# Expert products in units of 256 slots, with operands split into two fp32r parts and the second weight split during the first product

## What is computed

```python
# x: 3072 tokens of 384; w1: [8, 384, 1024]; w2: [8, 1024, 384]
do_compute = x @ w_skip > 0
xc = x[do_compute]
logits = xc @ w_gate
e_idx = np.argmax(logits, axis=1)
...
for e in range(E):
    mask = e_idx == e
    h = np.maximum(xc[mask] @ w1[e], 0.0)
    y[mask] = gate_w[mask, None] * (h @ w2[e])
out[do_compute] = xc + y
```

## Time and profile before

| | us |
|---|---|
| median of 3 runs (lowest, highest) | 1186.78 (1181.9, 1187.18) |
| profiled execution | 1180.28 |
| its span | 1178.5 |
| attention, to the first instruction of routing | about 441 |
| routing | 441 to 471 |
| experts, to the first load of `gated` | 471 to 696.6 |
| gated | 696.6 to 1178.5 |

### The profile page before, as it was taken

One profiled execution on the slowest core, in us unless ns is written; L12 is line 12 of the kernel. 1 busy time (PEld: TensorE's weight loads), 2 busy tenths in 40 slices (PEclk: granted clock), 3 DMA queues, 4 the chain that ended last, 5 costly groups with the idle time before them and its releaser, 6 DMA issues. The chain is left out here.

```text
span 1178.5 us, 23738 instructions
## 1 busy us (share of the span) xinstructions
PE 943.0 (80%) x10039; PEld 785.7 (67%) x10040; DVE 442.5 (38%) x808; ACT 282.0 (24%) x527; POOL 85.9 (7%) x113
## 2 busy tenths in 40 slices
PE   0239508885699983599999929999999999999997
PEld 0139407885688882255555518888888888888886
DVE  4762593359457117112121115542232232322322
ACT  2113202332133330011111124532323223223221
POOL 1301100102000000121112200000000000000000
PEclk9998656777589785799999968999999999999999
DMA  9203200331123115633454120001020010100101
GB/s 245 53 1 83 81 0 16 83 93 46 42 70 93 44 47 214 261 140 140 155 196 164 40 67 28 1 16 39 1 54 1 1 54 0 27 0 0 28 1 27
DMA packets 26164, 78.06 MB, mean 66 GB/s; under 512 B 4224, under 2 KB 16640, under 8 KB 23648
## 3 DMA queue, kind: packets, MB, share of 16 engines
q1 hardware_dynamic: 23904, 70.12, 18.6%
q0 software_dynamic: 2176, 6.69, 1.8%
HBM read 59.49 MB, written 17.30 MB: 65 GB/s over the span
## 5 line engine op out<-in xcount | busy, mean ns | idle before, releaser
L1212 PE MATMUL pg<-xT,wg 128*128 128x512 f32 x648 | 164.8, 398 | 1.8 <-DVE xT L1144 1.8
L1196 PE MATMUL po<-wo,hh 128*128 128x384 f32 x864 | 163.7, 337 | 0.1
L1212 PE MATMUL pv<-xT,wv 128*128 128x512 f32 x648 | 158.7, 389 | 0.0
L1196 PEld LDWEIGHTS po<-wo,hh 128*128 128x128 f32 x864 | 153.2, 188 | 5.6 <-DVE hh L1156 0.4
L1212 PEld LDWEIGHTS pv<-xT,wv 128*128 128x128 f32 x648 | 121.7, 188 | 26.2
L1212 PEld LDWEIGHTS pg<-xT,wg 128*128 128x128 f32 x648 | 121.1, 190 | 26.5 <-DVE xT L1144 3.0
L1154 DVE TENSOR_TENSOR hf<-pv,sil 128x512 f32<-128x512 f32 x72 | 49.8, 692 | 226.7 <-PE pv L1212 200.7
L940 PE MATMUL ph<-w1s,xgT 128*128 x192 | 87.8, 608 | 3.2 <-issue 3.2
L445 PE MATMUL pzx<-T,Q 32*32 32x32 f32 x768 | 16.5, 203 | 86.1 <-DVE T L363 52.9
L958 PE MATMUL py<-w2s,hT 128*128 x256 | 85.2, 486 | 0.0
L1103 ACT CAST hh<-hf 128x512 fp32r<-128x512 f32 x72 | 44.8, 622 | 151.4 <-DVE hf L1154 151.4
(11 more groups left out here) (183 smaller groups left out, 1049.2 us busy)
## 6 DMA issues: line engine op xcount, KB each, us to landing
w1s<-in_w SPq DMA_DIRECT2D x8, 1536.0 KB, 6.7
w2s<-in_w SPq DMA_DIRECT2D x8, 1536.0 KB, 10.5
kT<-in_kT SPq DMA_DIRECT2D x24, 192.0 KB, 6.2
ktok<-in_ktok SPq DMA_DIRECT2D x12, 384.0 KB, 7.4
qT<-in_qT SPq DMA_DIRECT2D x24, 192.0 KB, 3.7
vt<-in_vtok SPq DMA_DIRECT2D x12, 384.0 KB, 5.8
x_gather<-xs SPq DMA_DIRECT2D x24, 192.0 KB, 1.9
x_next<-xs SPq DMA_DIRECT2D x24, 192.0 KB, 2.0
```

The lines of the kernel that those rows point to most:

```text
L1196: ins = nc.tensor.matmul(po[j][:, 0:DM], a[:, j * 128:(j + 1) * 128], w[:, f, :], start=(f == 0 and n == 0), stop=(f == K2 - 1 and n == 2))
L1212: ins = nc.tensor.matmul(ps[:], a[:, k, c], x[:, k, :], start=(k == 0 and n == 0), stop=(k == KD - 1 and n == 2))
```

## The change

The padding is now to 256 slots, so `routing` makes units of 256 (2 tiles of gather and scatter indices each), RT is 40, and the table holds only the expert of each unit and the number of pairs of units. `experts` loops over pairs of units (10 passes at most). For each unit, whether its expert is new or not, both weights are loaded into a single buffer each and split on the chip: ACT writes `w1h[0]`, `w2h[0]` (hi), DVE writes `w1h[1]`, `w2h[1]` (lo), in halves of 1536 columns. The tokens are split into `xh`, the hidden values into `hh`. The first product has w1 as the stationary operand, so the hidden values come out with the hidden dimension on the partitions and the 8 transposes, `phT` and `hT` go. It is 72 fp32r matmuls of 256 columns; the second is 48 of 384 columns. The halves of the w2 split stand in ACT's and DVE's programs among the four groups of the first product, the split of the next unit's w1 behind the last group. `xr` goes; `yo` reads `xg`, so a gather into `xg` waits for the `yo` of the unit before the last.

```diff
--- before.py
+++ after.py
...
+UNIT = 256
+MAXU = 20
+RT = 2 * MAXU
...
-            remainder(pad[:, 1], pad[:, 0], 128)
...
+            remainder(pad[:, 1], pad[:, 0], UNIT)
...
-            for e in range(2, E):
-
-                sp.wait_ge(s_w[e % 2], 16 * NWL * (e // 2))
-                sp.wait_ge(s_y, reg(sp, TAB_ENDS + e - 2, 1, RT + 1))
...
+
+            def body(t, b, i):
+                e = reg(sp, TAB_EXPERT + t + 1, 0, E - 1)
+                sp.wait_ge(s_c1l, t + 1)
+                sp.wait_ge(s_c1h, t + 1)
+                sp.dma_start(w1s[:], w1_d[bass.ds(e, 1)].rearrange("o p n -> p (o n)")).then_inc(s_w1, 16)
+                sp.wait_ge(s_c2l, t + 1)
+                sp.wait_ge(s_c2h, t * 2 + 2)
+                sp.dma_start(w2s[:], w2_d[bass.ds(e, 1)].rearrange("o p n -> p (o n)")).then_inc(s_w2, 16)
...
             def gather(t, b):
...
+                for j in range(2):
+                    nc.gpsimd.tensor_copy(gi[b][j][:], gidx[:, bass.ds(t * 2 + j, 1)]).then_inc(s_gi, 1)
+                pool.wait_ge(s_gi, t * 2 + 2)
                 pool.sem_inc(s_step, 1)
-                nc.gpsimd.indirect_dma_start(out=xg[b][:], out_offset=None, in_=x_gather_d,
-                                             in_offset=bass.IndirectOffsetOnAxis(ap=gi[b][:, 0:1], axis=0)
-                                             ).then_inc(s_g[b], 16)
+                for j in range(2):
+                    nc.gpsimd.indirect_dma_start(out=xg[b][:, j], out_offset=None, in_=x_gather_d,
+                                                 in_offset=bass.IndirectOffsetOnAxis(ap=gi[b][j][:, 0:1], axis=0)
+                                                 ).then_inc(s_g[b], 16)
...
             def scatter(t, b, i):
...
+                for j in range(2):
+                    pool.wait_ge(s_yo, t * 2 + j + 3)
+                    pool.sem_inc(s_step, 1)
+                    nc.gpsimd.indirect_dma_start(out=x_next_d,
+                                                 out_offset=bass.IndirectOffsetOnAxis(ap=si[b][j][:, 0:1], axis=0),
+                                                 in_=yo[b][:, j], in_offset=None).then_inc(s_st[b], 16)
+
+            gather(0, 0)
+            gather(1, 1)
+
+            def body(t, b, i):
+                scatter(t, b, i)
+                gather(t + 2, b)
+                pool.wait_ge(s_st[b], i * 32 + 32)
...
-            def body(t, b, i):
-                gather(t + 2, b)
-                scatter(t, b, i)
-            pairs = tiles(pool, body)
...
+            def w1_hi(t, half):
+                c = slice(half * W1 // 2, (half + 1) * W1 // 2)
+                ins = nc.scalar.copy(w1h[0][:, c], w1s[:, c])
+                if half:
+                    ins.then_inc(s_c1h, 1)
+
+            def w2_hi(t, half):
+                c = slice(half * W2 // 2, (half + 1) * W2 // 2)
+                ins = nc.scalar.copy(w2h[0][:, c], w2s[:, c])
+                ins.then_inc(s_c2h, 1)
+
+            def x_hi(t, b):
                 act.wait_ge(s_xT, t + 1)
-                nc.scalar.copy(xgT[b][:].rearrange("p k n -> p (k n)"), pxT[:, 0:DM]).then_inc(s_xTe, 1)
+                nc.scalar.copy(xh[b][0][:, 0:2].rearrange("p k n -> p (k n)"), px[0][:])
+                nc.scalar.copy(xh[b][0][:, 2], px[1][:, 0:UNIT]).then_inc(s_xhi, 1)
 
             def body(t, b, i):
-                for f in range(2):
-                    act.wait_ge(s_h, t * 2 + f + 1)
-                    nc.scalar.activation(h[b][:, f * 512:(f + 1) * 512], ph[f][:], ACT.Relu).then_inc(s_he, 1)
+                act.wait_ge(s_w2, t * 16 + 16)
+                act.wait_ge(s_py, t * 2 + 2)
+                w2_hi(t, 0)
+                for f in range(4):
+                    act.wait_ge(s_ph, t * 4 + f + 1)
+                    nc.scalar.activation(hh[0][:, 2 * f:2 * f + 2].rearrange("p k n -> p (k n)"), ph[f][:],
+                                         ACT.Relu).then_inc(s_hhi, 1)
                     if f == 0:
-                        transposed(t + 1, 1 - b)
-            transposed(0, 0)
-            tiles(act, body)
+                        w2_hi(t, 1)
+                x_hi(t + 1, 1 - b)
+                act.wait_ge(s_w1, t * 16 + 32)
+                for half in range(2):
+                    w1_hi(t + 1, half)
+            act.sem_inc(s_py, 2)
+            act.wait_ge(s_w1, 16)
+            for half in range(2):
+                w1_hi(0, half)
+            x_hi(0, 0)
...
-            def keep(t, b, i):
-                dve.wait_ge(s_g[b], i * 16 + 16)
-
-                dve.wait_ge(s_yo, t + 1)
-                nc.vector.tensor_copy(xr[b][:], xg[b][:]).then_inc(s_xr, 1)
...
+            def w1_lo(t, half):
+                c = slice(half * W1 // 2, (half + 1) * W1 // 2)
+                ins = v.tensor_tensor(w1h[1][:, c], w1s[:, c], w1h[0][:, c].bitcast(F32), ALU.subtract)
+                if half:
+                    ins.then_inc(s_c1l, 1)
+
+            def w2_lo(t, half):
+                c = slice(half * W2 // 2, (half + 1) * W2 // 2)
+                ins = v.tensor_tensor(w2h[1][:, c], w2s[:, c], w2h[0][:, c].bitcast(F32), ALU.subtract)
+                if half:
+                    ins.then_inc(s_c2l, 1)
+
+            def x_lo(t, b):
+                dve.wait_ge(s_xhi, t + 1)
+                v.tensor_tensor(xh[b][1][:, 0:2].rearrange("p k n -> p (k n)"), px[0][:],
+                                xh[b][0][:, 0:2].rearrange("p k n -> p (k n)").bitcast(F32), ALU.subtract)
+                v.tensor_tensor(xh[b][1][:, 2], px[1][:, 0:UNIT], xh[b][0][:, 2].bitcast(F32),
+                                ALU.subtract).then_inc(s_xlo, 1)
 
             def body(t, b, i):
-                keep(t + 1, 1 - b, i + b)
-                for f in range(2):
-                    dve.wait_ge(s_hT, t * 2 + f + 1)
-                    nc.vector.tensor_copy(hT[b][:, f * 4:f * 4 + 4, :].rearrange("p k n -> p (k n)"),
-                                          phT[f][:]).then_inc(s_hTe, 1)
-
-
-                dve.wait_ge(s_y, t + 2)
-                dve.wait_ge(s_xr, t + 2)
-                nc.vector.scalar_tensor_tensor(out=yo[b][:], in0=py[b][:, 0:DM], scalar=gate[:, bass.ds(t, 1)],
-                                               in1=xr[b][:], op0=ALU.mult, op1=ALU.add).then_inc(s_yo, 1)
-            keep(0, 0, 0)
-            tiles(dve, body)
+                for f in range(4):
+                    dve.wait_ge(s_hhi, t * 4 + f + 1)
+                    k = slice(2 * f, 2 * f + 2)
+                    v.scalar_tensor_tensor(out=hh[1][:, k].rearrange("p k n -> p (k n)"), in0=ph[f][:], scalar=0.0,
+                                           in1=hh[0][:, k].rearrange("p k n -> p (k n)").bitcast(F32),
+                                           op0=ALU.max, op1=ALU.subtract).then_inc(s_hlo, 1)
+                    if f < 2:
+                        dve.wait_ge(s_c2h, t * 2 + f + 1)
+                        w2_lo(t, f)
+                x_lo(t + 1, 1 - b)
+                dve.wait_ge(s_c1h, t + 2)
+                for half in range(2):
+                    w1_lo(t + 1, half)
+                for j in range(2):
+                    dve.wait_ge(s_py, t * 2 + j + 3)
+                    dve.wait_ge(s_free, t + 1)
+                    v.scalar_tensor_tensor(out=yo[b][:, j], in0=py[j][:, 0:DM], scalar=gate[:, bass.ds(t * 2 + j, 1)],
+                                           in1=xg[b][:, j], op0=ALU.mult, op1=ALU.add).then_inc(s_yo, 1)
+            dve.wait_ge(s_c1h, 1)
+            for half in range(2):
+                w1_lo(0, half)
+            x_lo(0, 0)
+            units(dve, body)
...
             def body(t, b, i):
...
-                pe.wait_ge(s_xTe, t + 2)
-                for f in range(2):
-                    pe.wait_ge(s_he, t * 2 + f + 1)
-                    for k in range(KD):
-                        ins = nc.tensor.matmul(ph[f][:], xgT[b][:, k, :],
-                                               w1s[:, bass.ds(slot, 1), k * F1 + f * 512:k * F1 + (f + 1) * 512
...
+                pe.wait_ge(s_c1l, t + 1)
+                pe.wait_ge(s_xlo, t + 1)
+                for f in range(4):
+                    for j in range(2):
+                        m = slice((2 * f + j) * 128, (2 * f + j + 1) * 128)
+                        for k in range(KD):
+                            w = slice(k * F1 + m.start, k * F1 + m.stop)
+                            for n, (a, x) in enumerate(((0, 0), (0, 1), (1, 0))):
+                                ins = nc.tensor.matmul(ph[f][:, j * UNIT:(j + 1) * UNIT], w1h[a][:, w],
+                                                       xh[b][x][:, k], start=(k == 0 and n == 0),
+                                                       stop=(k == KD - 1 and n == 2))
+                    ins.then_inc(s_ph, 1)
                 transpose_x(t + 1, 1 - b, i + b)
-                for f in range(2):
-                    pe.wait_ge(s_he, t * 2 + f + 3)
-                    pe.wait_ge(s_hTe, t * 2 + f + 1)
```

(45 more changed lines are left out.)

164 lines of the change are left out of this document (62 added, 102 removed).

## The result

The changed kernel is **not faster but 0.9% slower**: 1193.45 us in the median (1190.92 to 1198.83, 8 runs) against 1186.58 (1178.4 to 1187.53, 8 runs), a ratio of 1.0088, 95% interval 1.006 to 1.0116. The interval excludes no change, but the difference is small, under 2%. The forecast was 1137, with a range from 1125 to 1168.

A forecast was written before the change was run, and what follows sets the result against it. PE was taken to bound the experts: first product at 490.3, 2.8 us cold and 8 units of 18.1 us brought gated 46 us earlier, giving 1134 or 1141, taken as 1137 us; range 1125 to 1168.

The forecast's parts named there:

- How many units: Experts stage: 8 units of 256 slots, one per expert, in 4 pairs, for 16 tiles before.
- PE's work in a unit: PE in the experts: a unit takes 18.1 us against 24.7 for two tiles, 53 us less for 8 units.
- rival (c): PE's 256-column matmuls: weight loads not hidden, 0.217 us per matmul, +53 us, so 1190; chance 0.05.
- The split of w1: ACT and DVE under the second product: 8.6 us plus 0.1 against 9.1 of cover, hidden by 0.4 us.
- rival (b): Split of w1: chain longer than its 0.4 us slack; 2 us more per unit is +16, 1153; chance 0.12.
- The split of w2: ACT and DVE under the first product: done at 8.2 us, PE wants it at 9.7; cost nothing.
- Ends of the stage: Experts' start and end: routing +2.5 us, first product 6.0 us later at 490.3, +1 us behind the last yo.
- the sum: Whole experts stage: the terms added up to gated at 650.5 for 696.6, 46 us less; 1137 taken.
- POOL: Gather queue: second gather issued at 4.9, landing at 8.2 us, 0.8 us before PE needs it; cost nothing.
- (a): Gathers late because DVE's w2 splits hold POOL: 1 to 2.5 us per unit, +8 to +20, up to +47; chance 0.20.

The follow-up runs named there:

- e1: Changed kernel with the xr copy back, so the gathers for unit t+2 stand ahead of the scatters of unit t; 1131.52 us.
- e10: Changed kernel with each half of DVE's w2 split as four instructions of 384 columns, same work in the same place; 1135.86 us.
- e3: Changed kernel with DVE's two halves of the w2 split behind the third and fourth hidden group instead of the first and second; 1155.21 us.
- e2: Changed kernel with SP waiting for the next unit's gathers to land before it loads the next w2; 1151.95 us.
- e7: e3 plus a spare 1.5 MB load that nobody reads, at the time of the changed kernel's w2 load; 1156.99 us.
- e4: Changed kernel with 24 filler matmuls of the identity on PE between the first product and the transposes; 1183.24 us.
- e11: Changed kernel with each half of DVE's w2 split as twelve instructions of 128 columns, same work in the same place; 1140.32 us.
- e8: e1 with gated's three 2.3 MB weight loads issued behind the w1 loads of the first two units; 1130.19 us.

## Why the prediction was wrong

**What held.** *How many units*: 8. *PE's work in a unit*: 17.6 us in e1 for 18.1; a matmul of 256 columns is 0.120 us (0.125 forecast), and rival (c), the weight loads in series at 0.217, is out. *The split of w1*: slack of 1.1 us for 0.4 (the two DVE halves took 3.4 us for 3.5, ACT's 2.9 for 3.1), so rival (b) is out. *The split of w2*: done 7.6 us into the unit for 8.2. *Ends of the stage*: from routing's start to the first product 47.4 us for 48.9 (of it routing 0.5 us more than before, forecast 2.5), from the last `yo` to `gated` 12.1 for 12.3; the cold first unit of 19.8 us is 2.2 over e1's others, for 2.8. e10, which keeps every order of the change, measures 1135.9 where the sum gave 1137; that it is so near is in part luck, since its unit of 18.1 us is 17.6 of work and 0.5 of waiting for the gathers.

**The step that failed** is *POOL*: "the second is issued at 4.9. A gather lands 3.3 us after issue in the median". The issue does start there where nothing holds it (5.2 in e3), but with DVE's splits it starts at 6.5 and ends at 8.4, and the gather is there only near 15: 8.6 us from its issue's start, for 3.3. The trace of before showed gathers only beside short DVE work; the row that spoke of long work was the earlier trace rows, and it was given to the rival.

**The rival was right in kind and mis-sized** in (a). It let POOL wait for one split; both issues are held, by 1.4 and 0.95 us. It let the second gather land at 10 to 11.5 "into the w2 load, 1 to 2.5 us late", as if landing beside the load cost little; e2 and e7 show that 2.2 us come from the hold, and 4.2 more from being issued behind the load. Its far end, "+47" from the 10.0 us landing of the earlier trace rows, came near the 6.5 us per unit, by other terms: 4.9 + 10.0 us there, 6.5 + 8.6 measured. The range left it out as the unlikely end. That row was a gather issued at 473.85, 2 us behind the last of `gated`'s three loads, and what the change made is a gather behind a large load: it was the nearest row, and the median was not.

**The term that was missing** is PE's clock. The sum priced each us of waiting as one us. The waits of 6.5 us put 1.6 us on the second product and 0.6 on the transposes: a unit is 8.7 us longer than in e1 (26.35 for 17.62), 6.5 of it waiting and 2.2 the clock; e4 gave back 2.3. Together 8.7 x 7 = 61 us, where the medians of e1 and the changed kernel lie 61.9 apart.

The Trainium skill (SBUF — State Buffer, "Who interferes with whom") has the lock for a whole instruction that the prediction set beside rival (a); the trace agrees for the gathers (1.75 us splits, 2.37 and 1.92 us issues; 1.16 with 0.5 us ones), and e11's second issue goes beyond it. The same section infers that a `tensor_tensor` leaves the generation of descriptors alone; here `tensor_tensor` is what held the issues of the gathers, so the measurement decides against that inference.

## What to carry to other kernels

When a change puts wide two-input VectorE work beside GpSimd's DMA issues, count each issue as waiting for the end of the instruction that runs, then look at what is issued in that time: a large load that gets ahead of a gather costs more than the hold. Cut such work into instructions of about half a microsecond (here 3 lines, 58 us), or move the gathers to where their data is not yet due. Many much shorter ones (0.2 us, e11) were no better. And price a wait of TensorE with the slower clock behind it: here a wait lengthened a unit by between 1.0 (e3) and 1.5 (e2) times its own length.

## What the runs showed of the hardware that I had not expected

- One SP load of 1.5 MB issued 0.7 us ahead of the end of a gather's issue went first: for 3 us none of the gather's 64 packets moved, and the tokens were ready 4.2 us later than without it (e2). Issued 1.3 us behind the end (e7), it delayed them by at most 0.4 us.
- Scatters were not seen held: 0.97 to 1.02 us throughout, though none of them lay beside a wide split. Index copies were: the two in e8 at 541.33 took 2.54 us, for 0.30, beside the splits of w1, and those of e11 took up to 1.7 us for 0.17.
- In e2, PE's waits before the transposes are 1.7 to 2.4 us long. Behind four of the seven (units 2, 3, 6 and 7) the second product was slow (9.4 to 10.0 us to the next first product, granted clock 0.84 in units 2 and 6), behind the other three it ran at full pace (8.4 us, clock 1.00 in units 4 and 5). A wait of 2.6 us between the transposes and the second product (e3) was followed by full pace as well. What decides, no run here shows.
- With every wait in the units gone, the granted clock stays at 1.00 through whole units (e1: PE busy 17.60 of 17.60 us).
